# Two weight loads issued at other steps of the SyncE queue of an attention and mixture-of-experts kernel

## The reference

```python
q_bits = (np.einsum('bhsd,dk->bhsk', q, proj) > 0)
mask = q_bucket[:, :, :, None] == k_bucket[:, :, None, :]
scores = np.where(mask, scale * np.matmul(q, k.transpose(0, 1, 3, 2)), -1e9)
attn = np.exp(scores - scores.max(-1, keepdims=True))
attn = attn / (attn.sum(-1, keepdims=True) + 1e-09)
x = np.matmul(attn, v)
```

## Time and profile before

| | |
|---|---|
| median of 3 runs | 733.06 us (732.15 to 733.19) |
| the profiled execution's own time | 733.19 us |
| its span, from the first to the last instruction | 731.4 us |
| mean granted TensorE clock, share of full speed | 0.993 |
| attention, from the start | about 225 us |

### The profile page before, as it was taken

One profiled execution on the slowest core, in us unless ns is written; L12 is line 12 of the kernel. 1 busy time (PEld: TensorE's weight loads), 2 busy tenths in 40 slices (PEclk: granted clock), 3 DMA queues, 4 the chain that ended last, 5 costly groups with the idle time before them and its releaser, 6 DMA issues. The chain is left out here.

```text
span 731.4 us, 13094 instructions
## 1 busy us (share of the span) xinstructions
PE 709.3 (97%) x4028; PEld 603.4 (83%) x4028; DVE 557.8 (76%) x897; ACT 488.6 (67%) x919; POOL 328.4 (45%) x303
## 2 busy tenths in 40 slices
PE   7999999999999979999999999999999999999996
PEld 4999999999998768888888878788887888878884
DVE  8999999989997556449991262588878788887874
ACT  7888888878887545459982464566566566566562
POOL 7986886788722710000000000255545845557543
PEclk9999999999999989999999999999999999999999
DMA  4215412132063484249990000123232432224221
GB/s 136 73 40 173 164 39 58 49 122 73 19 231 115 135 287 142 90 141 344 345 376 1 0 29 0 56 92 112 86 96 92 159 101 100 86 89 170 86 82 61
DMA packets 40530, 85.05 MB, mean 116 GB/s; under 512 B 5584, under 2 KB 9840, under 8 KB 40496
## 3 DMA queue, kind: packets, MB, share of 16 engines
q1 hardware_dynamic: 37776, 77.01, 31.2%
q0 software_dynamic: 2000, 6.98, 2.9%
q10 hardware_dynamic: 720, 0.64, 0.3%
HBM read 76.82 MB, written 6.68 MB: 114 GB/s over the span
## 5 line engine op out<-in xcount | busy, mean ns | idle before, releaser
L606 POOL TENSOR_TENSOR hres<-hexp,hres 128x512 f32<-128x512 f32 x46 | 59.9, 1303 | 306.9 <-DVE hres L1338 210.2
L678 ACT ACTIVATE pTh<-psA 128x384 fp32r<-128x384 f32 x192 | 83.8, 490 | 36.3 <-PE psA L1416 34.8
L966 DVE TENSOR_TENSOR pTl<-psA,pTh 128x384 fp32r<-128x384 f32 x192 | 97.9, 551 | 11.1 <-ACT pTh L678 9.6
L959 DVE TENSOR_SCALAR_CACHE_REDUCE psA<-psA 128x768 f32<-128x768 f32 x96 | 91.8, 956 | 1.7 <-PE psA L1410 1.6
L1410 PE MATMUL psA<-K,Q 128*128 128x384 f32 x384 | 89.9, 356 | 2.5 <-ACT probs L662 1.6
L662 ACT ACTIVATE probs<-psA,negmax 128x768 f32<-128x768 f32 x96 | 87.3, 910 | 0.4 <-DVE psA L959 0.4
L877 ACT ACTIVATE habs<-psA 128x512 f32<-128x512 f32 x48 | 28.7, 598 | 79.1 <-PE psA L1689 79.0
L1244 DVE TENSOR_TENSOR wil<-rawi,wih 128x512 fp32r<-128x512 f32 x48 | 77.5, 1617 | 0.0
L609 POOL TENSOR_TENSOR hsum<-hsum,hres 128x512 f32<-128x512 f32 x46 | 69.5, 1512 | 10.1 <-POOL hres L606 8.7
L1228 DVE SCALAR_TENSOR_TENSOR hTl<-psA,hTh 128x512 fp32r<-128x512 f32 x32 | 21.9, 686 | 67.5 <-ACT hTh L783 67.5
L1707 PE MATMUL psA<-woh,sl 128*128 128x512 f32 x184 | 71.7, 390 | 1.0 <-DVE sl L1317 1.0
(11 more groups left out here) (249 smaller groups left out, 1688.6 us busy)
## 6 DMA issues: line engine op xcount, KB each, us to landing
w2s<-in_moe_w SPq DMA_DIRECT2D x9, 2048.0 KB, 8.8
w1s<-in_moe_w SPq DMA_DIRECT2D x9, 2048.0 KB, 7.8
rawi<-in_moe_w_in SPq DMA_DIRECT2D x48, 256.0 KB, 2.6
rawo<-in_moe_w_out SPq DMA_DIRECT2D x48, 256.0 KB, 2.7
raw<-in_qk SPq DMA_DIRECT2D x16, 384.0 KB, 3.1
vs<-in_v SPq DMA_DIRECT2D x16, 192.0 KB, 2.4
x_rows<-X SPq DMA_DIRECT2D x1, 1728.0 KB, 6.4
x_rows<-X SPq DMA_DIRECT2D x1, 1512.0 KB, 5.6
```

What stands on the lines that cost most here:

```text
L678: nc.scalar.activation(pTh[u // TPGR % 2][:, g * TPH:(g + 1) * TPH, u % TPGR * P:(u % TPGR + 1) * P], psA[2][:, g, 0:HALF].rearrange("p (t ...
L959: V.tensor_scalar(psA[u % 2][:, :, 0:HALF], psA[u % 2][:, :, 0:HALF], PENALTY, PENALTY, ALU.min, ALU.min, accum_out=negmax[:, u % 4:u % 4 ...
L966: V.tensor_tensor(pTl[u // TPGR % 2][:, g * TPH:(g + 1) * TPH, cols], psA[2][:, g, 0:HALF].rearrange("p (t n) -> p t n", t=TPH), pTh[u // ...
```

## The change

The two weight loads of expert 0 are issued at i = 2 and i = 3 of the loop and no longer at i = 6 and i = 7. An even i issues `load_w2(0)`, an odd i `load_w1(0)`, as before. Nothing else differs.

```diff
@@ -391,7 +391,7 @@
                 if i > 2:
                     load_raw(i, i % 2)
                 load_v(i, i % 2)
-                if 5 < i < 8:
+                if i < 4:
                     (load_w2, load_w1)[i % 2](0)
                 if i == H + 5:
                     sp.wait_ge(bias0_ready, 1)
```

## The result

| | before | changed |
|---|---|---|
| median of 6 runs each | 732.79 us | 737.76 us |
| lowest and highest | 732.15 to 733.19 | 735.57 to 739.05 |
| ratio, 95% interval | | 1.0061 (1.0042 to 1.0082) |
| span of the profiled execution | 731.4 us | 729.6 us |

The change costs 5.0 us by the medians (3.1 to 6.0 by the interval). I had forecast 735.1 us, 2.0 us over the kernel before, with a range from 733.2 to 736.4 us: the right sign, and too small by 3 us. Sixteen further executions of the changed kernel, with none of the kernel before beside them, took 734.75 to 740.23 us.

What follows compares the result with a forecast made beforehand. The prediction took a full TensorE (97% busy) as the bound. Contention netted to nothing and a 2.0 us wait for head 2's bits was added: 733.06 + 2.0 = 735.1 us, range 733.2 to 736.4 us.

Steps and rivals of the forecast that it cites:

- Where TensorE is bound: From 20 to 35 us TensorE has no idle time, so each microsecond it waits is one at the end.
- w2 at i = 2 harms nothing: Issued near 16.42 us, w2 lands at 25.7, raw of head 3 at 26.8 us, 1.7 us before its first reader.
- The bits of head 2 wait behind w1: On SyncE's queue they land at 33.4 us, due at 31.44, so TensorE waits 2.0 us; chance of 1.5 to 3: 0.63.
- the bits behind w1: Eight transfers of bits for head 2 on SyncE's queue, put at 0.43 us after w1 lands at 32.9 us.
- I let a wait of TensorE cost its own length: At head 2's scores, the 2.0 us wait was added to the total as 2.0 us, with no later cost.
- Contention of 0.25 us: The loads cost 0.25 us beside attention at their old places and the same at the new; net nothing.
- the third (SyncE slowed by what is queued): Bits of head 2 issue at 1.4 us each, giving a wait of 3.5 us and 736.6 us; chance 0.05.
- The first (bits overtake): Bits of head 2 land by 31.44 us despite w1, TensorE never waits, 733.1 us; chance 0.12 together with the fourth.
- the fourth: Less contention without the cost, the first heads hiding the transfers: 732.8 us; chance 0.12 together with the first.
- The second (a quicker queue, a wait of 1.0 us): SyncE's queue keeps order but runs faster, so head 2's scores wait 1.0 us, 734.1 us; chance 0.2.

Runs made afterwards that it cites:

- Experiment 1: Changed kernel with only w2 issued early (i = 2) and w1 at its old place; 731.91 us against 732.55 us, ratio 0.9993.
- experiment 3: Changed kernel with both loads early, but w1 issued behind the eight transfers of bits of head 2; 732.5 against 732.55 us, ratio 1.0002.
- Experiment 8: Changed kernel with both early loads issued by ScalarE on its own queue instead of SyncE's; 729.62 against 725.43 us, ratio 1.0059.
- experiment 11: Only w1 early, issued by ScalarE on its own queue, w2 at its old place; 733.52 against 732.43 us, ratio 1.0018.
- three quarters: Changed kernel with three quarters of w1 (1536 KB) issued at i = 3, the last quarter at i = 7; 727.06 against 725.43 us, ratio 1.0034.
- experiment 2: Changed kernel with only w1 issued early (i = 3) and w2 at its old place; 734.21 against 732.55 us, ratio 1.0026.
- experiment 5: Changed kernel unaltered, run and profiled again on a chip where the kernel before took 725.43 us; 730.65 us, ratio 1.0077.
- experiment 9: Changed kernel unaltered once more, on a chip where the kernel before took 732.43 us; 736.15 us, ratio 1.0061.
- the filled kernel: Changed kernel plus 14 matmuls of ones on TensorE before its wait for the bits of head 2; run twice: 736.9 us (ratio 1.0052) and 736.81 us (1.0062).
- experiment 7: Changed kernel with one half of w1 (1024 KB) issued at i = 3, the rest at i = 7; 725.92 us, ratio 1.0005.

## Why the prediction was wrong, step by step

- **Where TensorE is bound**: right. In 20 to 35 us it was full, and nothing of the loss was caught up: 5.98 us at head 3, 5.9 us at the end of attention.
- **w2 at i = 2 harms nothing**: right. I had w2 at 25.7, raw at 26.8 us; they landed at 26.3 and 27.3 us, and the hash of head 3 did not move. Experiment 1 shows it alone.
- **The bits of head 2 wait behind w1**: right in effect. The landings come in order, and experiment 3 removes the whole loss by that order alone. But I ascribed it to the one queue, and experiments 8 and 11 show that a large load on the other queue holds them as well. The Trainium skill (DMA: Bandwidth & Descriptors, section Queues, rings and completion order) says that each engine takes turns between the queues that have work, packet by packet. By that I would expect the bits to come ahead of a large load on the other queue. Experiment 8 agrees in part (TensorE was let go at 34.31, w1 landed at 36.0 us); in experiment 11 TensorE was let go at 33.58 us, 0.6 us after w1's landing and 0.7 us later than behind w1 on one queue. These runs don't tell why.
- **The first term that was mis-sized**: the bits behind w1. I put down 0.43 us from their engine time; from w1's landing to TensorE's start it took 1.4 us in the first profile of the changed kernel and with three quarters, 1.7 us in experiments 2 and 5, and 1.15 us in experiment 9. With w2 0.6 us later and w1's step 0.2 us longer than taken, the wait was 3.3 us in the first two profiles instead of 2.0 (the scores 3.5 us late in the first); in the third it was 2.6 us.
- **The step that was missing**: I let a wait of TensorE cost its own length. In two of three profiles of the changed kernel the clock fell to half behind it and cost another 2.5 us (50.99 - 45.01 - 3.51) and 1.6 us (49.73 - 34.58 = 15.15 against 13.57). Worked out from windows of half a microsecond, the clock was low for 6.8 us in the first (33.8 to 40.6) and for 3.3 us in the second (34.8 to 38.1). In experiment 11 it was low for 3.4 us (33.8 to 37.2) and again cost 1.6 us (48.73 - 33.58 = 15.15). In the first and in experiment 11 the clock fell during the wait, in the second just behind it (its wait ended at 34.58 us). The kernel before had shown it: TensorE nearly idle from 256 to 261 us, then 0.57 of the clock in 260 to 265 us. I had not read that stretch, since the change does not touch it.
- **Contention of 0.25 us**: wrong. With the loads gone from there, the changed kernel still takes 78.28 - 64.54 = 13.74 us from head 4 to head 5, as before (13.77); experiment 3 takes 13.72. The 0.2 us belong to that place in the program, not to w2.
- **The rivals**: the third (SyncE slowed by what is queued) did not occur; the bits took their usual 3.04 and 2.98 us to issue. The first (bits overtake) is excluded by the wait that ends with them, and with it the fourth. The second (a quicker queue, a wait of 1.0 us) did not occur either: w1 landed 0.7 us later than in my sum, and not 0.5 us earlier.

Wait plus clock, 3.3 + 2.5 us, make the 5.8 to 6.0 us that attention lost in the first profile, and 2.6 + 0 the 2.7 us of the third; the medians of 5.0, 5.2 and 3.7 us over the kernel before lie between. What decides from execution to execution whether the clock falls is open: it fell after 1.95, 3.25 and 3.30 us of idle time and not after 1.26, 1.40, 2.61 and 2.65 us. Between 30 and 45 us it fell in no profile without such a wait, nor in the two with the wait filled; but the filled kernel was profiled only twice, and one of three profiles of the unfilled one shows no fall either, so that the idle time is the cause rests on the mean clocks as much as on the profiles. Open too is why one chip has the gather wait and another has not.

## What to carry to other kernels

Before a large load is moved up a queue, ask which small transfer stands behind it and when that one is due; "the engines are mostly idle" is an average, and what counts are the bytes in flight at that moment. The cure here was order: the same load behind the small ones cost nothing, and a second queue left most of the loss (4.2 of 5.2 us with both loads, 1.1 of 1.7 us with w1). And price a new wait of a full TensorE not at its length alone but with a possible stretch at half clock behind it: here 0 to 2.5 us more.

## What the runs showed of the hardware that I had not expected

- The kernel before takes 725.4 us on one chip and 732.5 us on another, and the 7 us are one wait in the gathers with the half clock that follows it: from the first transposes of the expert stage to the first product with w2h it takes 37.9 us in experiment 1 and 31.3 us in experiment 7, where attention ends as in the kernel before. A profile of one and a profile of the other can be compared stage by stage only.
- A 192 KB load took 6.6 us (2.4 in the median of all) beside a 2 MB load, and later a second one behind it, on another issuing engine's queue. On SyncE's own queue behind w2 alone it took 5.2 us (experiment 1).
- While the last of twelve gathers ran (255 to 260 us, DMA share 0.80), matmuls without any dependence started 1.4 us apart.
